# Laying decay and carry rows over the partitions: one-hot products on TensorE in place of broadcast reads through DRAM

## The reference, cut to what matters

```python
m_new = np.maximum(f_gate[:, :, t] + m, i_gate[:, :, t])
f_stab = np.exp(f_gate[:, :, t] + m - m_new)
i_stab = np.exp(i_gate[:, :, t] - m_new)
C = f_stab * C + i_stab * np.einsum('bhd,bhe->bhde', vt, kt)
n = f_stab * n + i_stab * kt
h_tilde = np.einsum('bhde,bhe->bhd', C, qt)
denom = np.maximum(np.abs(n . q), 1.0)
y = sigmoid(o_gate) * h_tilde / denom
```

## Time and profile before

| | us |
|---|---|
| median of 3 runs (780.43 to 789.48) | 788.5 |
| the profiled execution | 785.55 |
| span of its trace | 783.8 |
| attention: from the span's start to the last write of X (L689) | 113.4 |
| router and mixtures: the rest | 670.4 |

### The profile page before, as it was taken

The page is one execution under the profiler, slowest core; times in us unless marked ns, Lnnn a source line. Parts: engine busy times, 40 slices in busy tenths (PEclk is TensorE's granted clock), DMA queues, the critical chain, the costliest instruction groups (busy, mean ns, idle before and its releaser), DMA issues.

```text
span 783.8 us, 11233 instructions
## 1 busy us (share of the span) xinstructions
PE 681.1 (87%) x3964; PEld 611.0 (78%) x3965; DVE 388.7 (50%) x601; ACT 287.2 (37%) x462; POOL 122.4 (16%) x140
## 2 busy tenths in 40 slices
PE   3587785229999999999956999999999999999997
PEld 2576672219989889889945899898988988898987
DVE  4434544936554536545514554555554554544522
ACT  4255324015544435435412433433332432432411
POOL 5433430460110110010014010011010000000000
PEclk9788987558999999999986999999999999999999
DMA  7998976076554545544017523423433423423000
GB/s 235 214 214 222 216 205 243 10 190 198 151 152 129 147 126 163 173 103 146 33 53 201 180 87 94 145 90 114 138 111 96 119 78 97 148 82 100 0 0 33
DMA packets 36211, 102.62 MB, mean 131 GB/s; under 512 B 5392, under 2 KB 15376, under 8 KB 36176
## 3 DMA queue, kind: packets, MB, share of 16 engines
q1 hardware_dynamic: 28688, 85.76, 38.9%
q0 software_dynamic: 3264, 11.15, 5.5%
q10 hardware_dynamic: 4224, 5.24, 1.8%
HBM read 88.93 MB, written 13.21 MB: 130 GB/s over the span
## 4 chain that ended last, share of the span: by engine, by line
PE 73%; DMA 9%; DVE 6%; issue 4%; ACT 2%; POOL 2%; SPq 1%; ACTq 1%; DVEq 0%; POOLq 0%
PE pY L1050 11%; PE pY L1052 11%; PE pY L1051 11%; PE pH L1037 9%; PE pH L1038 9%; PE pH L1039 8%; DMA E<-decay_rows 6%; PE pH L1042 4%; PE pH L1040 4%; PE pT L1018 2%; ACT E L518 1%; PE psF L982 1%; DVE h_lo L824 1%; DVE in_row L778 1%; PE pT L1019 1%
## 5 line engine op out<-in xcount | busy, mean ns | idle before, releaser
L562 ACT ACTIVATE h_hi<-pH 128x512 fp32r<-128x512 f32 x160 | 95.8, 599 | 296.1 <-PE pH L1042 292.1
L824 DVE SCALAR_TENSOR_TENSOR h_lo<-pH,h_hi 128x512 fp32r<-128x512 f32 x160 | 110.4, 691 | 180.6 <-ACT h_hi L562 175.4
L1050 PE MATMUL pY<-w_hi,h_hi 128*128 128x320 f32 x608 | 189.0, 311 | 4.1 <-DVE h_lo L824 3.7
L1052 PE MATMUL pY<-w_hi,h_lo 128*128 128x320 f32 x608 | 187.5, 308 | 0.0
L1051 PE MATMUL pY<-w_lo,h_hi 128*128 128x320 f32 x608 | 187.5, 308 | 0.0
L1037 PE MATMUL pH<-x_hi,w_hi 128*128 128x512 f32 (+2 forms) x324 | 128.1, 395 | 14.0 <-issue 12.6
L1038 PE MATMUL pH<-x_lo,w_hi 128*128 128x512 f32 (+2 forms) x324 | 124.7, 385 | 0.0
L1050 PEld LDWEIGHTS pY<-w_hi,h_hi 128*128 128x128 f32 x608 | 114.2, 188 | 13.0 <-issue 7.6
L1039 PE MATMUL pH<-x_hi,w_lo 128*128 128x512 f32 (+2 forms) x324 | 124.2, 383 | 0.0
L653 DVE TENSOR_TENSOR w_lo<-stage,w_hi 128x1024 fp32r<-128x1024 f32 (+1 forms) x80 | 108.5, 1358 | 25.8 <-ACT w_hi L507 25.8
L1051 PEld LDWEIGHTS pY<-w_lo,h_hi 128*128 128x128 f32 x608 | 114.3, 188 | 4.2
(11 more groups left out here) (164 smaller groups left out, 600.9 us busy)
## 6 DMA issues: line engine op xcount, KB each, us to landing
stage<-in_w SPq DMA_DIRECT2D x40, 640.0 KB, 3.9
stage<-in_w SPq DMA_DIRECT2D x40, 512.0 KB, 3.6
stage<-in_w SPq DMA_DIRECT2D x40, 256.0 KB, 3.8
E<-decay_rows SPq DMA_DIRECT2D x16, 384.0 KB, 12.3
results_by_slot<-acc ACTq DMA_DIRECT2D x8, 640.0 KB, 3.5
qk<-in_qk_t SPq DMA_DIRECT2D x16, 240.0 KB
kv<-in_kv_n SPq DMA_DIRECT2D x8, 480.0 KB
results_by_slot<-acc SPq DMA_DIRECT2D x6, 640.0 KB, 8.8
```

The lines of the kernel that those rows point to most:

```text
L562: act.activation(HH[s % 2][:, :], pH[s % 2][:, :], ACT.Relu).then_inc(hh_done[layer], 1)
L824: dve.scalar_tensor_tensor(out=HL[s % 2][:, :], in0=pH[s % 2][:, :], scalar=0.0, in1=f32(HH[s % 2][:, :]), op0=ALU.max, op1=ALU.subtract). ...
L1050: pe.matmul(y[:, 0:XD], hh, wh, start=(f == 0), stop=False)
L1052: return pe.matmul(y[:, 0:XD], hl, wh, start=False, stop=(f == NF - 1))
```

## The change

The DRAM tensors, `load_decays`, `load_carries` and the tile `gb` go. `dc` and `gr` are each split into a rounded part (float32r, copied by ACT) on partitions 0 to 15 and the rest (a subtraction on DVE) on partitions 32 to 47 of `decay_rows` and `carry_rows`, whose other partitions POOL zeroes. `picks` has a one at partitions n and 32+n of column n; used as the stationary operand, repeated over 128 columns (`pick`) or 64 (`pick_wide`), it makes a product that lays row n over all partitions, in PSUM. `decays(i)` does this for the two heads of a pair with four products of 512, 256, 256 and 512 columns into `psD` (3 banks), `carries(i)` with two products of 512 and 256 columns into the first half of the same `psD`. Eight small products before the first pair give the chunk-end carries of all pairs (`chunk_end`), which `states` uses. `psS` has one buffer in place of two.

ACT's exp reads psD and writes `E`. The product `qg = q * carry` moves from POOL to DVE (`carried`), first in its work for a pair. The order of PE for pair i becomes: chunk sums, decays(i+1), PM times v1, scores(i+1), carries(i+1), qg times C. Both halves of the sigmoid come after pair 1 of ACT. All loops over the pairs are written out. The order of the first loads changes: pair 0, half the output gates, pair 1, the other half.

```diff
-        psS = [pb(f"psS{n}", [P, CH, 2, P], att_ps) for n in range(2)]
+        psS = pb("psS", [P, CH, 2, P], att_ps)
+        psD = pb("psD", [P, 2 * S], att_ps)
@@ sync
-            def load_decays(i, par, h):
-            def load_carries(i, par):
-            def next_pair(i, par):
+            for i in range(2):
+                sp.wait_ge(pads, 2 * i + 2)
+                load_transposed(i, i)
+                load_by_position(i, i)
+                load_output_gates(i * OG, (i + 1) * OG)
+            for i in range(2, PAIRS):
                 sp.wait_ge(s_mm, i - 1)
                 sp.wait_ge(qg_done, i - 1)
+                load_transposed(i, i % 2)
                 sp.wait_ge(v1_done, i - 1)
+                sp.wait_ge(dc_mm, i - 1)
+                load_by_position(i, i % 2)
@@ gpsimd
+            for tile in (decay_rows, carry_rows):
+                pool.memset(f32(tile[:, :]), 0.0).then_inc(rows_zero, 1)
+            pool.memset(picks[:, :], 0.0).then_inc(sel_built, 1)
+            for n in range(2):
+                pool.wait_ge(sel_built, n + 1)
+                pool.affine_select(out=picks[:, :], in_=picks[:, :], compare_op=ALU.not_equal, fill=1.0, base=-32 * n,
+                                   pattern=[[-1, BH]], channel_multiplier=1).then_inc(sel_built, 1)
...
-                    pool.wait_ge(att_y, i + 1)
-                    pool.wait_ge(carry_in[par], 32 * j + 32)
-                    pool.tensor_tensor(qg[par][:, :], qT[par], gb[par][:, :], ALU.mult).then_inc(qg_done, 1)
@@ scalar
+            act.wait_ge(sel_built, 3)
+            act.activation(pick[:, :], picks[:, :], ACT.Copy).then_inc(sel_ready, 1)
+            act.activation(pick_wide[:, :, :], picks[:, :].unsqueeze(2).to_broadcast([P, BH, HB]), ACT.Copy).then_inc(sel_ready, 1)
+            act.wait_ge(rows_zero, 2)
+            act.wait_ge(decay_ready, 1)
+            act.activation(decay_rows[0:BH, :], dc[:, :], ACT.Copy).then_inc(decay_hi, 1)
+            act.wait_ge(carry_sum, 1)
+            act.activation(gr[:, :], gr[:, :], ACT.Exp).then_inc(carry_ready, 1)
+            act.wait_ge(carry_ready, 1)
+            act.activation(carry_rows[0:BH, :], gr[:, :], ACT.Copy).then_inc(carry_hi, 1)
...
+                act.wait_ge(decay_mm, i + 1)
                 for h in range(2):
+                    if i >= 2:
+                        act.wait_ge(pm_done, 2 * (i - 2) + h + 1)
                     for c in range(CH):
+                        ins = act.activation(E[par][:, h, c, :], psD[:, h * S + c * P:h * S + (c + 1) * P], ACT.Exp,
+                                             bias=acol[:, c, 2 * i + h:2 * i + h + 1])
                     ins.then_inc(exp_done, 1)
+                if i == 1:
+                    output_gates(0, OG)
                     output_gates(OG, PAIRS)
@@ vector
+            dve.wait_ge(decay_hi, 1)
+            dve.tensor_tensor(decay_rows[32:32 + BH, :], dc[:, :], f32(decay_rows[0:BH, :]), ALU.subtract).then_inc(decay_lo, 1)
...
+            dve.memset(psC[:, 0:2 * (CH - 1) * D1], 0.0).then_inc(state_zero, 1)
+            dve.wait_ge(carry_hi, 1)
+            dve.tensor_tensor(carry_rows[32:32 + BH, :], gr[:, :], f32(carry_rows[0:BH, :]), ALU.subtract).then_inc(carry_lo, 1)
+            dve.wait_ge(ends_mm, 1)
+            dve.tensor_copy(chunk_end[:, :, :], psC[:, 2 * CH * D1 - PAIRS * CH:2 * CH * D1].rearrange("p (i c) -> p i c", i=PAIRS)).then_inc(ends_ready, 1)
...
+            def carried(i, par):
+                dve.wait_ge(qk_in[par], 80 * (i // 2) + 80)
+                dve.wait_ge(carry_mm, i + 1)
+                if i >= 2:
+                    dve.wait_ge(att_y, i - 1)
+                dve.tensor_tensor(qg[par][:, :], qT[par], psD[:, 0:S], ALU.mult).then_inc(qg_done, 1)
...
+            for i in range(PAIRS):
+                par = i % 2
+                carried(i, par)
                 mults(i, par)
+                if i >= 1:
+                    if i == 1:
+                        dve.wait_ge(o_ready, 2)
                     outputs(i - 1)
+                states(i, par)
@@ tensor
+            def decays(i):
+                if i >= 1:
+                    pe.wait_ge(qg_done, i)
                 for h in range(2):
+                    who = pick[:, 2 * i + h:2 * i + h + 1].to_broadcast([P, P])
+                    for n0, n1 in (((0, 512), (512, S)), ((0, 256), (256, S)))[h]:
+                        ins = pe.matmul(psD[:, h * S + n0:h * S + n1], who, decay_rows[:, n0:n1], start=True, stop=True, skip_group_check=True)
+                ins.then_inc(decay_mm, 1)
+
+            def carries(i):
+                pe.wait_ge(exp_done, 2 * i + 2)
+                if i == 0:
+                    pe.wait_ge(carry_lo, 1)
+                who = pick_wide[:, 2 * i:2 * i + 2, :].rearrange("p h d -> p (h d)")
+                for n0, n1 in ((0, 512), (512, S)):
+                    ins = pe.matmul(psD[:, n0:n1], who, carry_rows[:, n0:n1], start=True, stop=True, skip_group_check=True)
+                ins.then_inc(carry_mm, 1)
...
+                    pe.wait_ge(c_done, i)
+                pe.wait_ge(vw_done, 2 * i + 2)
...
+                if i + 1 < PAIRS:
+                    decays(i + 1)
+                if i >= 1:
+                    pe.wait_ge(y_read, i)
...
+                if i + 1 < PAIRS:
+                    scores(i + 1, 1 - par)
+                    carries(i + 1)
```

More of the change, by code:

```diff
@@ L158, in build @@
         E = [sb(f"E{n}", [P, 2, CH, P], F32, att) for n in range(2)]
-        gb = [sb(f"gb{n}", [P, S], F32, att) for n in range(2)]
+        decay_rows, carry_rows = (sb(n, [P, S], F32R, att) for n in ("decay_rows", "carry_rows"))
+        picks = sb("picks", [P, BH], F32, att)
+        pick = sb("pick", [P, BH], F32R, att)
+        pick_wide = sb("pick_wide", [P, BH, HB], F32R, att)
+        chunk_end = sb("chunk_end", [P, PAIRS, CH], F32, att)
         PM = [sb(f"PM{n}", [P, 2, CH, P], F32, att) for n in range(2)]
@@ L421, in _ @@
             pool.iota(jeven[:, :, :], pattern=[[2, SLOTS // 2], [0, 2]], base=0, channel_multiplier=0, allow_small_or_imprecise_dtypes=True).then_inc(consts, 1)
[L423 to L436, removed]
-                    pool.wait_ge(att_y, i + 1)
-                    pool.wait_ge(carry_in[par], 32 * j + 32)
-                    pool.tensor_tensor(qg[par][:, :], qT[par], gb[par][:, :], ALU.mult).then_inc(qg_done, 1)
+            for i in range(PAIRS):
+                par = i % 2
+                pool.wait_ge(v1_done, i + 1)
+                if i >= 1:
+                    pool.wait_ge(dc_mm, i)
+                for h in range(2):
+                    pool.wait_ge(exp_done, 2 * i + h + 1)
+                    last = E[par][:, h, :, P - 1:P].to_broadcast([P, CH, D1])
+                    pool.tensor_tensor(vw[h][:, :, :], v1[par][:, :, h, :], last, ALU.mult).then_inc(vw_done, 1)
+                    pool.wait_ge(vw_done, 2 * i + h + 1)
+                    pool.affine_select(out=E[par][:, h, :, :], in_=E[par][:, h, :, :], compare_op=ALU.is_ge, fill=0.0, base=0,
+                                       pattern=[[0, CH], [1, P]], channel_multiplier=-1).then_inc(sel_done, 1)
             pool.wait_ge(x_done, 1)
@@ L931, in scores @@
                 for c in range(CH):
-                    ins = pe.matmul(psS[par][:, c].rearrange("p h t -> p (h t)"), kT[par][:, c * P:(c + 1) * P],
+                    ins = pe.matmul(psS[:, c].rearrange("p h t -> p (h t)"), kT[par][:, c * P:(c + 1) * P],
                                     qz[par][:, c].rearrange("p h t -> p (h t)"), start=True, stop=True, skip_group_check=True)
                 ins.then_inc(s_mm, 1)
-            def pair(i, j, par, last=False):
-                pe.wait_ge(c_done, i + 1)
+            def decays(i):
+                if i >= 1:
+                    pe.wait_ge(qg_done, i)
@@ L938, in pair @@
                 for h in range(2):
-                    pe.wait_ge(vw_done, 2 * i + h + 1)
-                    for c in range(CH - 1):
+                    who = pick[:, 2 * i + h:2 * i + h + 1].to_broadcast([P, P])
[10 more added lines that the diff above has]
+                ins.then_inc(carry_mm, 1)
@@ new lines, in _ @@
+            pe.wait_ge(sel_ready, 2)
+            pe.wait_ge(decay_lo, 1)
+            decays(0)
+            scores(0, 0)
+            pe.wait_ge(carry_lo, 1)
+            pe.wait_ge(state_zero, 1)
+            for i in range(PAIRS):
+                who = pick_wide[:, 2 * i:2 * i + 2, :].rearrange("p h d -> p (h d)")
+                ins = pe.matmul(psC[:, 2 * CH * D1 - (PAIRS - i) * CH:2 * CH * D1 - (PAIRS - i - 1) * CH], who, carry_rows[:, P - 1:S:P], start=True, stop=True, skip_group_check=True)
@@ L941, in pair @@
+            ins.then_inc(ends_mm, 1)
+            carries(0)
+            for i in range(PAIRS):
+                par = i % 2
+                if i == 0:
+                    pe.wait_ge(ends_ready, 1)
+                else:
+                    pe.wait_ge(c_done, i)
```

(9 more changed lines are left out.)

114 lines of the change are left out of this document (41 added, 73 removed).

## The result

Over 20 runs of each kernel the changed one takes 789.66 us (787.42 to 794.1) and the one before 784.62 us (778.74 to 789.48): ratio 1.0075, 95% interval 1.0051 to 1.0099. It is slower by 0.75%, where 8 us less were forecast. The profiled execution took 794.1 us, with a span of 792.2 us against 783.8.

What follows compares the result with a forecast made beforehand. Transfers were taken to bound the attention's pairs; a 10.15 us cycle put the last X at 103.0, 105.5 with 1 and 1.5 us added, 8 us less than now: 788.5 - 8 = 780.5, given as 780, 80% range 771 to 790.

Steps and rivals of the forecast that it cites:

- What bounds the kernel, and what goes away: In the pairs: transfers set the pace at 212 GB/s; 1152 of 2352 KB per pair go, leaving 5.8 us of loads.
- Prices on PE: Added PE products per pair: decays 0.9 us, carries 0.5; PE alone would need 9.1 us, waiting about 1 us a cycle.
- The ring: PE and DVE hand over in turn through single-buffered psD and psS; cycle 10.15 us per pair against 11.24.
- the allowances: Added to the last X at 103.0: 1 us for handovers, 1.5 us for products at the low clock, giving 105.5.
- The start: Before the pairs: POOL's additions +2.8 us, pair 0's loads landing near 15, first exp at 17.1 against 17.31 now.
- outputs(0) would about meet the sigmoids: First pair: sigmoids on ACT until about 35.6 us, outputs(0) otherwise starting at 34.5, taken as about met.
- The clock: PE in the pairs: high level (2.4 GHz) expected for most, with 1.5 us allowed for one or two falls.
- Rival B: PE's clock falls within every cycle: 2.9 us more per pair, cycle 13.0, last X at 128.6, 803 us; chance 0.07.
- Straight code "nothing": Written-out loops over the pairs: instruction fetch of straight code was given no cost, bounds 0 to 2 us.

Runs made afterwards that it cites:

- the variants of it that leave the attention's data path alone: The kernel before with its pair loops written out (786.79 us), or with 64 (788.51 us) or 128 (784.93 us) idle instructions added to PE's program in the router.
- The run with dense filler: The changed kernel with five products of 512 columns put into PE's wait for yt; 769.32 us, 0.981 of the kernel before.
- the run with the mended start: The changed kernel with scores(i+1) before the yt wait, pair 0's tiles zeroed first and PE's transposes waiting for the identity only; 766.93 us, 0.977 of the kernel before.

## Why the prediction was wrong

- **What bounds the kernel, and what goes away: right.** DMA share 0.49 in the pairs and no wait for loads after the second pair. That the attention of the kernel before differs so much between executions was missed: the variants of it that leave the attention's data path alone had the last X 4 to 6 us later (117.3 to 119.7) than the 113.4 I started from.
- **Prices on PE: right.** Decays 0.95 us (0.9 forecast), carries 0.6 to 0.7 (0.5), the new qg on DVE 0.95 (0.96). The exp from PSUM was shorter, 3.2 us for twelve in place of 3.6, and hidden. PE's own work in a cycle came to 8.79 us, where the prediction added 9.1, so at the high clock it waited 1.40 us and not about 1.
- **The ring: right at the high clock.** The run with dense filler has this ring without the clock's fall: 9.95 us a cycle (10.15 forecast), last X at 103.8 (103.0 before the allowances), of which 2.6 us are its one cycle that fell.
- **The start: right as a sum, wrong in its parts.** POOL's additions were 4.3 us, not 2.8: the two selects took 2.67 in all where I took 0.3 each. The constants still ended near 14.5, since the select for the identity shrank from 1.77 to 0.39. The traces show why in DVE's rows. Under the select of the identity in the kernel before (7.68 to 9.45) stood

```profile
7.61 1.75 DVE L638 TENSOR_TENSOR_SCAN dc<-reset,dd 16x768 f32<-16x768 f32 x1
```

and the select ended 0.1 us behind this scan. The same holds wherever a select ran beside an operation of the gate chain with two inputs that was already under way or began with it: it ended 0 to 0.2 us after it, at 1.62 and 0.90 us for the two of 128x16 in the changed kernel, 1.41 for the identity in the run with the mended start. The one that began ahead of such an operation, the first of 128x16 there, took 0.19. So 0.3 was fair for a select alone, and what was missed was the gate chain beside it. First exp at 17.92 (17.1 forecast), since pair 0's loads landed at 17.4 and not near 15. That outputs(0) would about meet the sigmoids was 1.4 us too kind: DVE waited 1.38 us for them, which is half of PE's 2.89 us in the second cycle.
- **The clock: the step that failed.** I read that a wait of about 1 us had left scores at the high level and gave 1.5 us for the low level in all. It was about 3 us in each cycle: PM times v1 3.8 us in the mean of the five cycles and scores to the start of carries 4.5, against 2.8 and 2.5, which is the 12.96 - 9.95 us between the changed kernel and the filled one. The row that showed 0.50 after light products and no long gap was the nearer one to the new cycle, and I set it aside. Its place in the kernel before, and that of a longer wait that did no harm:

```profile
96.48 2.86 PE L932 MATMUL psS<-qz,qk 128*128 128x256 f32 x12 [2.08 <-DMA kv<-in_kv_n]
...
106.12 3.01 PE L953 MATMUL psYa<-v,PM 128*128 128x41 f32 x24 [1.94 <-DVE yt L686]
```

After 2.08 us of waiting came the dense scores, and the clock stayed. After 1.94 us came PM times v1, and the clock fell before qg times C. The new ring puts a wait in front of PM times v1 in every cycle, so the second of these rows was the one to price it by. The rule of the Trainium skill that I quoted, of a clock that falls and rises in a ring over PSUM banks though no pause is long, forecast the fall rightly. Its ground, the short pauses, isn't enough by these runs: light products without a pause lost the clock too, and the same ring with dense products kept it.
- **Rival B was what happened.** Its cycle of 13.0 us was measured as 12.96, its place (PM times v1, scores) was right, and its last X, 128.6, came at 125.7: it counted eight falls of 2.9 us, and the trace has a first cycle of 8.28 us without one, a second of 16.4, and five of 12.96. It had a chance of 0.07. Its 803 us were 13 too many: 2.9 in the attention, 3.9 after it, 3.9 because it stood on a median of 788.5 where 20 runs gave 784.62, and the rest because the changed kernel's profiled execution was one of its longest. That the median, 789.66, still lies inside the stated range of 771 to 790 is luck: its upper end was meant for a ring that gains nothing, not for one that loses 12 us of attention in the trace and has part of that given back elsewhere.
- **Straight code "nothing": wrong, and of the other sign.** Written-out loops cost nothing in themselves (1.0014) and alone left the pause at 9.25 us, but the new length of PE's program as a whole shifted an instruction fetch off PE's path, 3.9 us net in the profile. Without it the change would have been slower by about 9 us rather than 5, an estimate from 5.0 + 3.9.

## What to carry to other kernels

When a change takes a kernel off its transfers and makes PE and DVE alternate, work out the cycle at both levels of PE's clock, and look in the old trace for stretches with light products, not only for long gaps: here the difference was 3 us in 10. A wait of PE in such a ring is best filled with dense work that is due anyway; moving scores one step ahead was worth 23 us. A pause with no releaser ahead of code behind a branch may be an instruction fetch: look for a packet of instructions in the queues just ahead of it, and shift the code with idle instructions before explaining it by the change.

## What the runs showed of the hardware that I had not expected

- PE's clock fell in every cycle of 13 us although PE waited 1.4 us of it, and again when light products of 40 columns filled that wait; with five products of 512 columns there (1.4 us) it never fell from the third qg to the last X. PM times v1, 24 instructions with a full weight load each, slowed from 2.8 to 5.15 us at the low level; the weight loads took 192 ns each in the mean at the high level and 320 at the low one.
- PE sat idle for 7 to 9 us ahead of a branched-to block, each time with one packet of instructions landing in a stretch in which weights and gathers filled the queues, and 128 idle instructions made it come or go.
- A DVE copy of 16x6 took 1.58 us beside one of POOL's memsets and 2.68 beside two, where it took 0.27 at best; POOL's selects ended with DVE's operation beside them, 0.39 to 1.77 us for one and the same 128x128.
